# An RWKV scan with a gated MLP and a channel mix: first pair turned like the others, last seven scan slots in a new order

## What is computed

```python
# 1. RWKV, 8 heads of 48, a state of 48 x 48 a head
for t in range(S):
    cur = einsum('bhd,bhe->bhde', u[None] * k[:, :, t], v[:, :, t])
    y[:, :, t] = einsum('bhd,bhde->bhe', r[:, :, t], state + cur)
    state = w[:, :, t, :, None] * state + einsum('bhd,bhe->bhde', k[:, :, t], v[:, :, t])
x = y.transpose(0, 2, 1, 3).reshape(B, S, 384)
# 2. gated MLP, tokens mixed by w_sg
h = gelu_tanh(x @ w_in)                       # 384 -> 1024
u_, v_ = h[..., :512], h[..., 512:]
v_n = (v_ - mean(v_)) / sqrt(var(v_) + 1e-6) * g_ln
x = x + (u_ * (einsum('ts,bsd->btd', w_sg, v_n) + b_sg[None, :, None])) @ w_out
# 3. channel mix with the token before
xk = mu_k * x + (1 - mu_k) * x_prev;  xr = mu_r * x + (1 - mu_r) * x_prev
out = sigmoid(xr @ w_r) * ((relu(xk @ w_k) ** 2) @ w_v)
```

## Time and profile before

| | us |
|---|---|
| median of 3 runs | 378.94 |
| lowest, highest | 372.89, 384.51 |
| the profiled execution | 377.46 |
| its span, first to last instruction | 375.7 |
| mean granted clock of TensorE | 0.973 |

### The profile page before, as it was taken

The page is one execution under the profiler, slowest core; times in us unless marked ns, Lnnn a source line. Parts: engine busy times, 40 slices in busy tenths (PEclk is TensorE's granted clock), DMA queues, the critical chain, the costliest instruction groups (busy, mean ns, idle before and its releaser), DMA issues.

```text
span 375.7 us, 11261 instructions
## 1 busy us (share of the span) xinstructions
PE 358.4 (95%) x4909; PEld 332.9 (89%) x4909; DVE 236.2 (63%) x399; ACT 180.4 (48%) x310; POOL 74.5 (20%) x113
## 2 busy tenths in 40 slices
PE   8997987988799999999999999999999999999996
PEld 6766776877697788999899999999999999999996
DVE  5898778888773789675453679788953116752111
ACT  4754667776644366621240682378648003754000
POOL 6860210221000000000000026039600001951000
PEclk9999899999856999999999999999999999999999
DMA  8587852334210231300000040150000111000011
GB/s 249 161 214 225 248 145 63 85 59 89 56 35 0 36 96 24 75 2 0 0 2 0 2 167 3 29 202 2 0 2 0 44 42 42 2 0 2 21 58 48
DMA packets 39568, 23.73 MB, mean 63 GB/s; under 512 B 25568, under 2 KB 39008, under 8 KB 39520
## 3 DMA queue, kind: packets, MB, share of 16 engines
q1 hardware_dynamic: 39104, 23.02, 22.1%
q10 hardware_dynamic: 416, 0.00, 0.1%
HBM read 18.29 MB, written 2.36 MB: 55 GB/s over the span
## 4 chain that ended last, share of the span: by engine, by line
PE 93%; issue 4%; ACT 1%; DVE 0%; ACTq 0%
PE ps L1308 22%; PE ps L1309 22%; PE ps L1310 21%; PE ps L1298 11%; PE ps L1222 5%; PE ps L1245 3%; PE ps L1277 2%; PE ps L1256 2%; PE ps L1227 2%; PE ps L1232 1%; PE ps L1218 1%; PE ps L1269 1%; ACT yT L754 1%; ACT uT L780 0%; ACT wT L713 0%
## 5 line engine op out<-in xcount | busy, mean ns | idle before, releaser
L1298 PEld LDWEIGHTS ps<-r,kT 48*64 48x64 f32 x1920 | 35.5, 141 | 15.4 <-issue 13.5
L682 POOL TENSOR_TENSOR sq_f<-sq_f 128x384 f32<-128x384 f32 x32 | 33.8, 1072 | 74.9 <-ACT sq_f L824 74.8
L1298 PE MATMUL ps<-r,kT 48*64 48x32 f32 x1920 | 40.2, 226 | 6.8 <-issue 6.7
L1118 DVE TENSOR_TENSOR ot<-ps,ee 128x384 f32<-128x384 f32 x12 | 6.7, 558 | 54.6 <-PE ps L1310 54.6
L951 DVE TENSOR_TENSOR kT<-kT,wb 112x384 f32<-112x384 f32 x40 | 22.5, 564 | 19.1 <-PE ps L1298 18.6
L1103 DVE TENSOR_TENSOR sq_l<-sq_f,sq_h 128x384 fp32r<-128x384 f32 x32 | 27.6, 864 | 10.4 <-ACT sq_h L829 10.4
L1310 PE MATMUL ps<-xk_h,wk_l 128*128 128x384 f32 x96 | 32.2, 335 | 0.0
L1309 PE MATMUL ps<-xk_l,wk_h 128*128 128x384 f32 x96 | 32.2, 335 | 0.0
L1308 PE MATMUL ps<-xk_h,wk_h 128*128 128x384 f32 x96 | 32.2, 335 | 0.0
L1308 PE MATMUL ps<-wv_h,sq_h 128*128 128x384 f32 x96 | 32.1, 334 | 0.0
L1310 PE MATMUL ps<-wv_h,sq_l 128*128 128x384 f32 x96 | 32.1, 334 | 0.0
(11 more groups left out here) (158 smaller groups left out, 899.3 us busy)
## 6 DMA issues: line engine op xcount, KB each, us to landing
vt<-in_v_dram SPq DMA_DIRECT2D x32, 72.0 KB, 2.8
sgn<-in_moe_w_sg_dram SPq DMA_DIRECT2D x18, 128.0 KB, 2.9
out_dram<-ot SPq DMA_DIRECT2D x12, 192.0 KB, 1.9
raw_w<-in_w_dram SPq DMA_DIRECT2D x7, 288.0 KB, 4.3
raw_k<-in_k_dram SPq DMA_DIRECT2D x7, 288.0 KB, 5.0
raw_r<-in_r_dram SPq DMA_DIRECT2D x7, 288.0 KB, 5.4
xT<-yT SPq DMA_DIRECT2D x24, 72.0 KB, 2.3
win_raw<-in_moe_w_in_dram SPq DMA_DIRECT2D x12, 128.0 KB, 4.3
```

The source lines that it names most:

```text
L682: nc.gpsimd.tensor_tensor(t, t, t, ALU.mult).then_inc(k_sq, 1)
L1298: ins = nc.tensor.matmul(to[CHUNK[g], (x * C + c) * cols:(x * C + c + 1) * cols], kU[lo:hi, s] if l == 0 else kT[q % 4][lo:hi, s], rU[lo:h ...
```

## The change

1. **Pair 0** goes the way of the others: it lands in a fourth set of `raw` tiles (over `win_h`), is laid into `tok` (k and w by DVE, r by ACT) and is turned by six transposes a kind. The r of pair 1 is laid by ACT too.
2. **u** comes in two loads of whole rows into `u_rows`, is transposed by PE into a PSUM bank behind k's first turn and copied by ACT into `ucol`; the first k and r copies wait for it.
3. **Clearing**: `aT` 0 and 1 by DVE, `aT` 2 and 3 by POOL behind slots 1 and 3.
4. **PE, slots 14 to 21**, in an order written out (`LAST`): one V group a slot from slot 15 to 20, U from slot 20 on. The two warming matmuls ahead of level 1 of pair 7 go.
5. **x_h and x_l of batch 0**: each block waits only for the pairs that it holds; ACT makes block 0 in slot 12, block 1 in slot 13, block 2 in slot 14; DVE makes all three low parts in slot 14. For that `bbc` and `gtmp` change places with `x_l`, the ring `sgn` is entered at another tile, and the load of `bbc` waits for the last sg turn.
6. **The norm**: statistics of V0 to V3 one a slot (16 to 19), those of V4 and V5 and the first half of `norm` at the head of slot 20, the second half and all six normalising steps at the head of slot 21, the six `vn_l` behind slot 21. The root is made on ACT in slot 20. The low halves of the weights move by one to three slots (two of w_sg, 4 and 5, to slot 21, w_out behind it).

```diff
     def pe_jobs(slot):
+        elif slot in LAST:
+            jobs = LAST[slot]
 ...
-            (2, 0): 1, (2, 1): 1, **{(q, 1): 2 for q in range(3, NP)}}
+            (2, 0): 1, (2, 1): 1, **{(q, 1): 2 for q in range(3, NP - 1)}}
-    EARLY_FIRST = {18: [("V", 0, 4)], 20: [("U", 0, 3)]}
-    EARLY_DENSE = {16: [("V", 0, 0), ("V", 0, 1)], 17: [("V", 0, 2), ("V", 0, 3)], 18: [("V", 0, 5)],
-                   19: [("U", 0, 0), ("U", 0, 1), ("U", 0, 2)], 20: [("U", 0, 4), ("U", 0, 5)],
-                   21: [("U", 0, 6), ("U", 0, 7)]}
-    ACT_LAST = {18: [("kt", 6), ("wm", 6), ("V", 0, 4), ("sy", 6), ("V", 0, 5)],
-                19: [("root", 0), ("y", 6), ("U", 0, 0), ("vn", 0), ("U", 0, 1), ("vn", 1), ("U", 0, 2), ("vn", 2)],
-                20: [("kt", 7), ("wm", 7), ("vn", 3), ("U", 0, 3), ("vn", 4), ("sy", 7), ("U", 0, 4), ("vn", 5), ("U", 0, 5)],
-                21: [("y", 7), ("U", 0, 6), ("U", 0, 7), ("high", 21)]}
+    LAST = {14: [("level", 5, 4), ("kt", 4), ("level", 6, 2), ("sg", 4), ("level", 7, 0), ("u", 4)],
+            15: [("level", 5, 5), ("sg", 5), ("level", 6, 3), ("yl", 4), ("V", 0, 0), ("level", 7, 1), ("y", 4)],
+            16: [("level", 6, 4), ("kt", 5), ("level", 7, 2), ("V", 0, 1), ("u", 5)],
+            17: [("level", 6, 5), ("level", 7, 3), ("V", 0, 2), ("yl", 5), ("y", 5)],
+            18: [("level", 7, 4), ("kt", 6), ("V", 0, 3), ("u", 6)],
+            19: [("level", 7, 5), ("V", 0, 4), ("yl", 6), ("y", 6)],
+            20: [("V", 0, 5), ("kt", 7), ("U", 0, 0), ("u", 7), ("U", 0, 1)],
+            21: [("yl", 7), ("U", 0, 2), ("y", 7)] + [("U", 0, n) for n in range(3, 2 * FT)]}
+    ACT_LAST = {14: [("kt", 4), ("wm", 4), ("sg", 4), ("high", 14), ("x", 2), ("sy", 4)],
+                15: [("sg", 5), ("high", 15), ("V", 0, 0), ("y", 4)],
+                16: [("kt", 5), ("wm", 5), ("V", 0, 1), ("high", 16), ("sy", 5)],
+                17: [("V", 0, 2), ("high", 17), ("y", 5)],
+                18: [("kt", 6), ("wm", 6), ("V", 0, 3), ("sy", 6)],
+                19: [("V", 0, 4), ("y", 6)],
+                20: [("V", 0, 5), ("kt", 7), ("wm", 7), ("root", 0), ("U", 0, 0), ("sy", 7), ("U", 0, 1)],
+                21: [("vn", 0), ("U", 0, 2), ("vn", 1), ("y", 7)]
+                    + [job for n in range(2, C) for job in (("vn", n), ("U", 0, n + 1))] + [("U", 0, 7), ("high", 21)]}
 ...
-                 ("sg", 0): 18, ("sg", 1): 18, ("sg", 2): 19, ("sg", 3): 20, ("sg", 4): 20, ("sg", 5): 21,
+                 ("sg", 0): 19, ("sg", 1): 19, ("sg", 2): 19, ("sg", 3): 19, ("sg", 4): 21, ("sg", 5): 21,
 ...
-            act.wait_ge(u_zeroed, 1)
-                for x, (lo, hi) in enumerate(HEADS):
-                    act.dma_start(ucol[lo:hi, :], u.rearrange("(a two) d -> two d a", two=2)[x]).then_inc(u_in, 16)
+            for x in range(2):
+                act.dma_start(u_rows[:, x, 0:D], u.rearrange("(a two) d -> two a d", two=2)[x]).then_inc(u_in, 16)
 ...
+            lay_rows(0, "r")
+            act.wait_ge(u_turned, 1)
+            nc.scalar.copy(ucol[0:ROWS, :], level_banks[0][0:ROWS, 1, 0:PPB]).then_inc(u_ready, 1)
             copy_turn(("k", 0))
+            copy_turn(("r", 0))
+            copy_turn(("w", 0))
+            lay_rows(1, "r")
             act.wait_ge(mask_step, 2 * LEVELS + 1)
             nc.scalar.copy(mask[CH:P, :, 0:CH // 2], ...)
-            copy_turn(("r", 0))
-            copy_turn(("w", 0))
 ...
             def high_x(b, m):
-                act.wait_ge(yt_stored, stored_at(PPB * (b + 1) - 1))
+                act.wait_ge(yt_stored, stored_at(PPB * b + min(((m + 1) * P - 1) // (2 * D), PPB - 1)))
 ...
-            second_pair("w")
+            first_rows("k", 0)
+            nc.vector.memset(aT[1][:, :, :, :], 0.0).then_inc(zeroed, 1)
+            first_rows("w", 0)
             dve.wait_ge(turned, turn_at[("r", 0)] + 1)
-            dve.wait_ge(u_in, 32)
+            dve.wait_ge(u_ready, 1)
             (the first rU copies, as before)
-            second_pair("k")
+            first_rows("w", 1)
+            first_rows("k", 1)
             first_k(0)
             first_r(0)
-            second_pair("r")
             for slot in range(SLOTS):
                 if slot == 20:
-                    apply_norm(0, range(3, 5))
+                    norm_stats(0, range(4, C))
+                    norm_begin(0)
+                if slot == 21:
+                    norm_end(0)
+                    normalise(0)
 ...
-                        if slot == 16:
-                            low_x(0, {4: 1, 2: 2}[l])
+                        if slot == 14 and l:
+                            low_x(0, {4: 0, 2: 1}[l])
 ...
+                if slot == 14:
+                    low_x(0, 2)
+                if 16 <= slot < 20:
+                    norm_stats(0, range(slot - 16, slot - 15))
+            low_vn(0)
 ...
                     for c in range(C):
-                        if q < LONG:
-                            for x, (lo, hi) in enumerate(((0, 64), (64, ROWS))):
-                                ins = nc.tensor.matmul(six_apart(dst[lo:hi], c), ..., ident[:, :], start=True, stop=True)
-                        else:
-                            ins = nc.tensor.transpose(...)
+                        ins = nc.tensor.transpose(six_apart(dst[0:ROWS], c), tok[q % TOKS][kind][:, c, 0:ROWS], ident[:, :])
 ...
             for job in FIRST_TURNS:
                 turn_job(job)
+                if job[0] == "k":
+                    pe.wait_ge(u_in, 32)
+                    pe.wait_ge(u_zeroed, 1)
+                    nc.tensor.transpose(level_banks[0][0:ROWS, 1, 0:PPB], u_rows..., ident[0:PPB, 0:PPB]).then_inc(u_turned, 1)
```

More of the change, by code:

```diff
@@ L57, in pe_jobs @@
             jobs = FILL[slot]
+        elif slot in LAST:
+            jobs = LAST[slot]
         elif slot % 2 == 0:
-            jobs = [("level", a - 2, 4), ("kt", a - 3)] + EARLY_FIRST.get(slot, [])
+            jobs = [("level", a - 2, 4), ("kt", a - 3)]
             jobs += [("level", a - 1, 2), ("w", a + 1)] + GATE.get(slot, [])
@@ L64, in pe_jobs @@
             jobs += GATE.get(slot, []) + [("y", a - 3)]
-        jobs = [job for job in jobs if 0 <= job[1] < NP]
-        return jobs + EARLY_DENSE.get(slot, [])
+        return [job for job in jobs if 0 <= job[1] < NP]
     def side_jobs(slot):
@@ L83, in act_jobs @@
         jobs = [job for job in jobs if job[0] == "high" or 0 <= job[1] < NP]
-        return jobs + EARLY_DENSE.get(slot, [])
+        return jobs + [("x", 0)] * (slot == 12) + [("x", 1)] * (slot == 13)
     FILL = {0: [("level", 0, 0), ("w", 1)],
@@ L241, in rwkv_gmlp_channel_mix_kernel @@
         ucol = down("ucol", [P, PPB], F32)
+        u_rows = down("u_rows", [PPB, 2, 64], F32)
         mask_first = down("mask_first", [P, P], I8)
@@ L438, in by_chunk, with raw_of @@
             return t.rearrange("d (c two t) -> d c two t", two=2, t=CH)
+        def raw_of(q):
+            return (q - 1) % RAWS if q else RAWS
         def in_rows(t):
@@ L883, in _ @@
                         copy_turn(job)
-                if slot == 14:
-                    for m in range(MT):
-                        high_x(0, m)
             for m in range(MT):
@@ L917, in _, with first_rows @@
             nc.vector.memset(ones[:, :], 1.0).then_inc(ones_made, 1)
[L918 removed]
+            nc.vector.memset(u_rows[:, :, D:64], 0.0).then_inc(u_zeroed, 1)
             for s in range(TOKS):
                 for x in "krw":
[L921 to L928 removed]
+                    nc.vector.memset(tok[s][x][:, :, D:64], 0.0).then_inc(zeroed, 1)
+            nc.vector.memset(aT[0][:, :, :, :], 0.0).then_inc(zeroed, 1)
+            def first_rows(kind, q):
+                dve.wait_ge(raw_in[raw_of(q)][kind], 16)
+                nc.vector.tensor_copy(in_rows(tok[q][kind][:, :, :]), by_token(raw[raw_of(q)][kind])).then_inc(first_rows_dve, 1)
             def first_k(q):
@@ L1040, in norm, with normalise, low_vn @@
                 nc.vector.tensor_tensor(lnrs[:, :], lnrs[:, :], lnt[:, :], ALU.mult).then_inc(ln_step, 1)
+            def normalise(b):
+                dve.wait_ge(ln_step, 8 * (b + 1))
+                for j in range(C):
+                    nc.vector.tensor_scalar(vv[:, j, :], vv[:, j, :], lnmv[:, j, 0:1], lnrs[:, j:j + 1],
+                                            ALU.subtract, ALU.mult).then_inc(vn_made, 1)
+            def low_vn(b):
+                for j in range(C):
+                    dve.wait_ge(vn_high, b * C + j + 1)
+                    nc.vector.tensor_tensor(vn_l[:, j, :], vv[:, j, :], vn_h[:, j, :].bitcast(F32),
+                                            ALU.subtract).then_inc(vn_low, 1)
             def apply_norm(b, js):
@@ L1320, in group_job @@
                 elif g < EARLY:
-                    turn_free([job for job in TURNS if turn_banks(job) is turn][-1])
+                    turn_free(("sg", C - 1))
                 if g == EARLY:
```

117 lines of the change are left out of this document (57 added, 60 removed).

## The result

| | before | after |
|---|---|---|
| median of 6 runs each, one chip | 374.84 | 369.73 |
| lowest, highest | 372.89, 384.51 | 368.18, 371.42 |
| the profiled execution | 377.46 | 370.64 |
| its span | 375.7 | 368.9 |
| mean granted clock of it | 0.973 | 0.981 |

A forecast was written before the change was run, and what follows sets the result against it. PE was taken to bound the kernel nearly all the way, stretched before the first G by an issue hole and half clock. Profiled 377.46 less 7.4 (late slots) and 0.4 (start) gave 369.7 us, range 363 to 378.

The forecast's parts named there:

- The clock in slots 14 to 21: V0 moved to slot 15 ends the half clock from about 101.5 to 118.5 us; 7.4 us won.
- E: Slots 15 to 20: half clock holds past V0, as V comes one group per slot; 28.6 us, 398; chance 0.06.
- B: Before V0 the clock is lost as long as before, in effect no change; 377.1 us; chance 0.22.
- 377.46 - 7.4 - 0.4: Whole kernel: profiled execution less the late stretch's clock gain and the start's gain, giving 369.7 us.
- The reason I named for the hole: PE's issue hole of 1.46 us at 99.07 fell while SP issued v loads, which stay.
- The start: Pair 0 turned by transposes: w copied at about 9.6 instead of 9.9; gain 0.4 us, bounds -2.0 to +1.0.
- Rival C: The start stays at half clock, k's 24 matmuls becoming a wait and six transposes; 372.5 us; chance 0.10.
- DVE in slots 14 to 21: PE's new waits on DVE work: 0.6 before V0 (1.2 with the issue hole), 1.3 in slot 20.
- the cover that I had at 0.9: Before the first G: DVE finishes normalising ahead of PE's last U, so G does not wait; 0.9 us spare.
- Rival D: Slots 18 to 21: DVE or ACT becomes the bound and the first G waits for vn_l; 372.5 us; chance 0.10.
- Idle time of 3.2: Slot 15 to the first G: PE's new waits and issue holes, 1.2 + 0.2 + 1.3 + 0.5 us.
- The clearings on POOL at 0: Early pairs: aT clearings moved to POOL cost nothing, covered by its slack; up to 1.6 us without cover.

## Why the prediction was right, and where it was not

**The clock in slots 14 to 21: held in the profiles, as said.** V0 follows the hole, and in ten of the eleven profiles with V0 in slot 15 the clock does not fall to 0.50 before G0; moved back, it is lost again. My size for it, 7.4, fits the profiled pair (7.6 for the stretch). E is not borne out: its clue would have been a clock below 1.00 between levels and single V groups. B is not either in these profiles, but over the runs it was half right: a usual run is at half clock as long as before, or longer (14.0 us against 10.5), only in the profiles not in this stretch.

**What failed is the median, and with it the clock as the cause of the gain in a usual run.** The step "377.46 - 7.4 - 0.4" took the profiled execution's lost clock for the usual one. It had 20 us at half clock where the median run had 10.5, so its 17 us in slots 15 to 18 were more than a usual run has to win, and the 7.4 / 17 = 0.44 a us that I paid is more than the 0.32 of the fit over the runs. 374.84 - 369.73 = 5.1 is what came, a ratio within 2% of 1, where I had given 0.54 to a gain over 2%. That the forecast of 369.7 was met to the last digit is luck in part. It follows from making the sum against the execution's own time (with the same gain off the median shown, 378.94, it would have been 371.1), and most of the 7.8 forecast was a lost clock that most runs don't have. The 5 us of a usual run came although the kernel after is at half clock no less. What gave them is shown in part only: the old order with most of its clock took 4.4 us more from y3 to G0, 2.6 of it idle time of PE, which my sum had growing (2.7 to 3.2) and not falling. With two profiles of the old order the division stays open.

**The reason I named for the hole was wrong.** I put it beside the v loads, whose issues were over at 98.52, half a us ahead of it. It stays with them gone, and it stands at PE's own instruction count and ends with a packet of its instruction queue.

**The start: the head of it right, the sum not.** I had the first level near 8.5; it is at 8.1, and at 7.7 to 8.8 in the other profiles. The 0.4 was for the span, and this came back with the other sign: 0.8 later at slot 15 in the profile. The step left out is the way from the first level to slot 15: the lead is 2.1 us at 22 us, and the 14 us at half clock from 30 on, which the profile before does not have at that place but for 3, take it back. Over the runs the new start costs nothing and gives nothing (1.002 alone), or little: 0.987 against 0.993 in one group, with intervals that overlap. With it the runs are at half clock some 4 to 5 us longer; at 0.3 a us that is 1 to 1.5 us, an estimate, a good part of the lead. Why it comes with the new start is not shown.

**Transposes run at full clock.** Six took 0.81 us for r at 6.08, right behind k's. Rival C is not borne out, nor what it shares with the rule of the Trainium skill ("TensorE: Matmul & The Clock Gate", Part 4: PE-mode transpose) that the full clock does not engage for transpose-mode work; by that rule, the trace does not agree.

**DVE in slots 14 to 21: walked in the right order, its waits too long.** V0 stands at 103.5, where I had 101.4. Of the 2.1 us, 0.8 is the later slot 15, 0.9 is idle time (1.49, all of it issue, where I had a wait of 0.6), and 0.4 is PE's work (3.73, where I had 3.3); the low parts ahead of the scan of pair 4 made PE wait for nothing there. The third `x_h` waited 1.30 us for its rows at 99.00, where I had the landing at 98.1, still ahead of what PE needed. In slot 20 the chain of the kernel after runs over DVE as said:

```profile
128.42 3.44 DVE wsg_l L1031 x4
131.86 1.80 DVE lnst L1045 x3
...
133.68 0.52 DVE lnmv L1051 x6
...
134.64 1.17 DVE sc L1020
...
136.18 0.89 PE ps L1295 x48
```

Four halves of w_sg, three statistics, the aggregates, then the scan that the last pair's states hang on. The four rows are 6.9 us by the trace, 3.44 + 1.80 where I had 3.8 + 2.0. PE waited 0.4 us, not 1.3, as the timeline has it:

```profile
136.18 0.89 PE L1295 MATMUL ps<-aT,vt 64*48 64x64 f32 x48 [0.38 <-DVE sy L1024]
...
145.70 0.69 DVE L1081 TENSOR_TENSOR vn_l<-vv,vn_h 128x512 fp32r<-128x512 f32 x1 [0.87 <-ACT vn_h L828]
```

The last `vn_l` ends at 146.39 and G stands at 147.5: the cover that I had at 0.9 is 1.1 us. Rival D is not borne out.

**The rest.** Idle time of 3.2 against 2.3 measured; PE's work 46.9 (3.73 + 43.20) where I had 46.2. The two errors nearly cancel: 49.4 and 49.2. The clearings on POOL at 0: right, in a stretch in which POOL is full.

## What to carry to other kernels

A dense group of matmuls put where PE tends to stall can keep its clock; leave it there and not behind the small work, and look where the stall goes if instructions are taken out. Before pricing a clock dip from one profile, hold that execution's time at half clock against that of all runs: it was twice the usual one here. After the change, compare runs with equal time at half clock: what is left between them is not the clock's, and here it was nearly the whole gain. An advance at the start is only worth what is left at the next common point, so measure it there and not where it arises.

## What the runs showed of the hardware

The long issue holes, up to 2.9 us, stand a multiple of about 252 PE instructions (matmuls and weight loads) apart, the distance of one 16.4 KB packet of the instruction queue. In 24 of 25 PE went on 1.3 to 1.7 us after such a packet had ended, and one of 1.1 us stood there with the DMA engines idle. Of the twenty of 1.2 us or more with no V group just behind them, fifteen went with a fall of the granted clock to 0.50, within the hole or up to 2.1 us behind it and for 3 to 17 us, though PE was busy 11.50 of 11.50 us in one such dip; five did not. With a V group just behind a hole of 1.1 to 1.4 us it did not fall in five profiles, behind 1.75 and 2.1 it did for 3.4 us. Nor did a drop need a long hole: in one profile the clock was at 0.50 from 25 us on, behind a hole of 0.60 at 24.0. Six transposes take 0.81 us at the full clock and 1.46 at half.
